# Attention outputs of units 4 to 23: their stores to HBM issued from ScalarE's queue in place of SyncE's

## The reference, cut to what matters

```python
def _attn_ref(q, k, v, alpha):               # batch 4, heads 8, seq 768, dim 48
    for t in range(S):
        state = alpha[:, :, t, :, None] * state + einsum('bhd,bhe->bhde', k[:, :, t], v[:, :, t])
        y[:, :, t] = einsum('bhd,bhde->bhe', q[:, :, t], state)

def _moe_ref(x, w_in, w_out):                # 3072 tokens, d_model 384, d_ff 2048
    h = x @ w_in
    return (h * (1.0 / (1.0 + np.exp(-1.702 * h)))) @ w_out

def _moe2_ref(x, w_in, w_out):               # the same sizes
    h = x @ w_in
    return (h - np.tanh(h)) @ w_out
```

## Time and profile before

| | |
|---|---|
| three runs | 967.51, 967.76, 970.03 us; median 967.76 |
| the profiled execution, its own time | 967.3 us |
| its span, first to last instruction | 965.5 us |
| granted TensorE clock, mean | 1.000 |
| busy: PE / DVE / ACT / POOL | 943.8 / 672.2 / 376.4 / 285.4 us |
| stores `attn_out<-y` from SPq | 92 of 48 KB, 1.8 us from issue to landing (median) |

### The profile page before, as it was taken

One profiled execution on the slowest core, in us unless ns is written; L12 is line 12 of the kernel. 1 busy time (PEld: TensorE's weight loads), 2 busy tenths in 40 slices (PEclk: granted clock), 3 DMA queues, 4 the chain that ended last, 5 costly groups with the idle time before them and its releaser, 6 DMA issues.

```text
span 965.5 us, 23370 instructions
## 1 busy us (share of the span) xinstructions
PE 943.8 (98%) x9705; PEld 830.0 (86%) x9705; DVE 672.2 (70%) x1615; ACT 376.4 (39%) x730; POOL 285.4 (30%) x314
## 2 busy tenths in 40 slices
PE   5899999999999999999999999999999999999998
PEld 4789999999999988888888888888888888888886
DVE  7879997878888877776322544357677677776765
ACT  1352333332332332333234664244444444444442
POOL 2666665646556554444001642000000000000000
PEclk9999999999999999999999999999999999999999
DMA  7943232423323332321113322010020020100101
GB/s 156 256 89 91 49 86 51 114 49 85 80 61 83 90 69 47 104 47 25 19 58 123 98 82 90 1 37 30 1 66 2 1 66 1 40 27 1 34 1 33
DMA packets 136234, 58.94 MB, mean 61 GB/s; under 512 B 114368, under 2 KB 131520, under 8 KB 136128
## 3 DMA queue, kind: packets, MB, share of 16 engines
q1 hardware_dynamic: 133488, 55.39, 22.8%
q10 hardware_dynamic: 2640, 2.05, 0.7%
HBM read 43.26 MB, written 13.96 MB: 59 GB/s over the span
## 4 chain that ended last, share of the span: by engine, by line
PE 92%; DVE 3%; DMA 2%; SPq 1%; POOL 1%; issue 1%; ACT 0%; DVEq 0%; POOLq 0%; ACTq 0%
PE pX L840 39%; PE pZ L864 16%; PE pX L864 9%; PE pZ L908 6%; PE pZ L914 6%; PE pX L908 4%; PE pX L704 3%; PE pZ L799 2%; PE pZ L732 2%; PE pZ L690 1%; PE pZ L742 1%; DMA k<-k_t 1%; PE pX L835 1%; PE pX L718 1%; PE pZ L790 1%; DVE scores L1212 1%
## 5 line engine op out<-in xcount | busy, mean ns | idle before, releaser
L840 PE MATMUL pX<-x_hi,w_hi 128*128 128x512 f32 (+2 forms) x624 | 227.7, 365 | 0.7 <-ACT g L1050 0.7
L840 PE MATMUL pX<-x_lo,w_hi 128*128 128x512 f32 (+2 forms) x624 | 227.3, 364 | 0.0
L840 PE MATMUL pX<-x_hi,w_lo 128*128 128x512 f32 (+2 forms) x624 | 227.3, 364 | 0.0
L1228 DVE TENSOR_TENSOR g_lo<-g,g_hi 128x512 fp32r<-128x512 f32 (+2 forms) x208 | 129.3, 637 | 87.5 <-ACT g_hi L1059 87.3
L1059 ACT ACTIVATE g_hi<-g 128x512 fp32r<-128x512 f32 (+2 forms) x208 | 121.3, 583 | 89.5 <-DVE g L1308 85.9
L1050 ACT ACTIVATE g<-pX 128x512 f32<-128x512 f32 (+3 forms) x144 | 65.7, 456 | 206.4 <-PE pX L840 173.2
L1308 DVE TENSOR_TENSOR g<-pX,sg 128x512 f32<-128x512 f32 x96 | 66.3, 690 | 106.2 <-ACT sg L1052 106.2
L840 PEld LDWEIGHTS pX<-x_hi,w_hi 128*128 128x128 f32 x624 | 117.5, 188 | 18.0 <-ACT g L1050 1.1
L840 PEld LDWEIGHTS pX<-x_lo,w_hi 128*128 128x128 f32 x624 | 117.5, 188 | 16.9
L840 PEld LDWEIGHTS pX<-x_hi,w_lo 128*128 128x128 f32 x624 | 117.5, 188 | 16.8
L596 POOL TENSOR_TENSOR r<-r,alpha 112x128 f32<-112x128 f32 (+2 forms) x115 | 109.5, 968 | 18.5 <-DMA r<-q_t 14.9
(11 more groups left out here) (166 smaller groups left out, 1899.4 us busy)
## 6 DMA issues: line engine op xcount, KB each, us to landing
v<-v_l SPq DMA_DIRECT2D x96, 48.0 KB, 2.6
x_raw<-hidden SPq DMA_DIRECT2D x6, 768.0 KB, 5.7
attn_out<-y SPq DMA_DIRECT2D x92, 48.0 KB, 1.8
out_t<-o SPq DMA_DIRECT2D x10, 384.0 KB, 3.5
alpha<-a_t SPq DMA_DIRECT2D x24, 128.0 KB, 2.9
r<-q_t SPq DMA_DIRECT2D x24, 128.0 KB, 3.0
k<-k_t SPq DMA_DIRECT2D x24, 128.0 KB, 3.0
w_raw<-w_in SPq DMA_DIRECT2D x16, 192.0 KB, 2.4
```

Of the source, the lines that this page charges most:

```text
L840: last = nc.tensor.matmul(pH(N)[:, 0:w], win(wp, f, m), XS[T % 2][xp][:, m, 0:w], start=(n == 0), stop=(n == len(terms) - 1))
L1228: nc.vector.tensor_tensor(at(GLs, N), g_raw(N), at(GHs, N).bitcast(F32), ALU.subtract).then_inc(gl_done, 1)
```

## The change

The SP loop keeps its wait and its stores only up to iteration 4 (units 1 to 3). From unit 4 on, ScalarE, having copied the second item of a unit, waits for that copy to have been written and issues the four stores itself. The waits of the other queues are unchanged. 80 of the 92 stores move, in 20 units. In the SP loop the values' load of unit U+1 now stands behind its own wait for `y_done` alone.

```diff
+        FROM_SP = 4
+
         def store_y(eng, U, batches=U2):
...
                 if U == 1:
                     sp.wait_ge(y_copied, 1)
                     first_inputs(sp, ((0, 0), (0, 1), (1, 0), (1, 1)))
-                sp.wait_ge(y_copied, 2 * U)
+                if U <= FROM_SP:
+                    sp.wait_ge(y_copied, 2 * U)
                 if U == 1:
                     first_inputs(sp, ((2, 0), (3, 0)))
-                else:
+                elif U <= FROM_SP:
                     store_y(sp, U - 1)
...
                 nc.scalar.activation(Y[U % 2][:, :, 2 * pp:2 * pp + 2, :], pY[buf(j)].rearrange("d (z q) t -> d z q t", z=2),
                                      ACT.Copy).then_inc(y_copied, 1)
+                if pp and U >= FROM_SP:
+                    act.wait_ge(y_copied, j + 1)
+                    store_y(act, U)
```

## The result

The changed kernel takes **980.25 us** (median; 978.87 to 981.96 over four runs) beside 968.89 us for the kernel before (967.51 to 970.03). The ratio is **1.0122, 95% interval 1.0108 to 1.0137**: 11.8 us slower by the ratio (the medians themselves lie 11.4 us apart). In a second comparison on another occasion it was 980.33 beside 968.47 us, 1.0123 (1.0098 to 1.0147). The forecast was 978 us, in a range of 969.5 to 986.

What follows compares the result with a forecast made beforehand. TensorE was taken to bound the kernel, its waits for the gelu adding 3.4 + 2.9 + 2.6 + 0.2 + 0.8 + 0.1 = 10.0 us to 967.8, so 978 us. The range was 969.5 to 986.

Steps and rivals of the forecast that it cites:

- What bounds the kernel: From unit 4 on TensorE always has work; faster loads or stores give back about 1 us at most, its waits add time.
- ScalarE is held by its issues: Ahead of the gelu, ScalarE stands idle for the whole length of its four issues, about 2.4 us in 20 units.
- D + 0.24 - room: TensorE's wait at odd items: D is the four issues' length, room the gelu-to-up(N+1) gap, 1.19 to 2.56 us; sum 10.0 us.
- D taken from SP's rows: ScalarE's four issues last as long as SP's did, unit by unit: 1.78 us at least, 2.65 to 3.02 in others.
- long ones: Sets of four store issues of 2.65 to 3.02 us instead of 1.78; twelve of the 20 units expected.
- q8 packet: A packet moved by the instruction queue within a unit's issues; long issues go with it, 1.78 us ones have none.
- Sharing with SP's queue: SP's values' loads run beside ScalarE's stores and lengthen issues by 0 to 7%, at most 1.5 us in all.
- The cover of VectorE and GpSimd: A later g_hi delays VectorE and GpSimd but is hidden, costed at nothing; without more cover 6 us, for the range.
- Rival 1: The prolonging sits in SP's sequencer; ScalarE issues in 1.78 us, leaving 2 us, 969.8 us in all; chance 0.15.
- Rival 2: SP's values' issues go between ScalarE's in 13 units: 23 us more, 33 in all, 1001 us; chance 0.08.
- Rival 3: With SP free, transfers come early and remove waits: at most 1.3 us gained, 967 us; chance 0.04.

Runs made afterwards that it cites:

- Experiments 1: The changed kernel, with ScalarE issuing the four stores behind g_hi of the same visit instead of ahead of the gelu: 970.63 us, 1.0017 of the kernel before.
- experiment 2: The kernel before, plus only ScalarE's wait for its own copy of y in the 20 units; SP still stores: 968.83 us, 0.9998 of the kernel before.
- experiment 6: The changed kernel measured once more, unchanged: 980.33 us, 1.0123 of the kernel before.
- experiment 5: The changed kernel, with each unit's output in eight stores of 24 KB instead of four of 48 KB: 1034.26 us, 1.0681 of the kernel before.
- experiment 4: The changed kernel, with ScalarE issuing two of a unit's four stores and SP the other two: 969.10 us, 0.9995 of the kernel before.
- experiment 7: The changed kernel, with ScalarE issuing two of each unit's four stores ahead of the gelu and two behind g_hi: 970.18 us, 1.0015 of the kernel before.

## Why the prediction was right, point by point

- **What bounds the kernel.** Right. SP now waits in other places (86.7 us for stores to land, where it waited 9.4), and nothing came of it, neither gain nor loss.
- **ScalarE is held by its issues.** Right: 44.9 us of idle put down to "issue" in 18 visits, 2.5 us each, against the 2.4 forecast. Experiments 1 and 2 separate it from ScalarE's queue as such and from the wait for the copy.
- **D + 0.24 - room.** Right in form, and its two hand-overs of 0.05 us are those of the chain above. Too small by 0.1 us at each of 14 visits: TensorE loses that beyond its wait. Of the 2.0 us between 10.0 forecast and 12.0 found, this is about 1.6, and other lengths D make the rest. The constant is the term of the sum that was mis-sized.
- **D taken from SP's rows.** Right on the whole: 20 units took 48.9 us on ScalarE, after 48.2 on SP. Each of the 11 long ones (2.48 us and more) again has a q8 packet that starts within it, and the eight in which none starts are at 1.79 to 2.25. Which units are hit is nearly the same as before: item 43 dropped out, item 9 came in (with a packet, but short). The place moves from run to run, the sum hardly. Item by item the agreement is in part luck: with the D of after, the 256 and 384 wide visits come out 1.1 us above the forecast and the 512 wide ones 0.9 us below. That no packet moved within a short one holds by the packets' starts alone: at items 17 and 23 one that had started earlier was still under way for 0.4 and 0.3 us of SP's issues.
- **Sharing with SP's queue.** Forecast as 0 to 7%, which was too little: it is 15% for most of the short ones, 0.27 us, and 26% at item 21. It matters only where the room is exceeded. There the issues under 0.7 us were longer than alone by 1.1 us in sum (1.4 in experiment 6), which is still under the 1.5 us that the range allowed; what sharing adds to a long issue can't be told apart.
- **The cover of VectorE and GpSimd.** Right. Over the same part of the program VectorE's waits for g_hi rose from 22.3 us (95 to 488 us before) to 45.4 (95 to 500 after), and TensorE's for scores fell. Even in experiment 5, with ScalarE late by 4 to 5 us, the profile has no wait of TensorE for scores, since TensorE was itself late.
- **Rival 1, the long issues are SP's own.** Fallen: ScalarE's are lengthened too.
- **Rival 2, one after another.** Fallen: 2.06 us beside SP's, not 3.7. With it falls, for this kernel, the reading that a whole issue locks the other queue out, which the Trainium skill ("Perfetto Trace Analysis", section "DMA Instruction — HWDGE (DVE, Sync)") suggests by its exclusive lock: the two queues' issues of 2.06 and 2.58 us ran over the same 2.7 us, where one after another they would take 4.4 (1.79 + 2.58). That a lock is held for a part of each issue is not excluded.
- **Rival 3, a gain.** Nothing of it in any run: the best of the variants, experiments 2 and 4, equal the kernel before. No version faster than the kernel before came out of this, and rows 1 and 2 say why: 1.3 us was all there was to gain.

What remains open is why an issue is longer when a q8 packet falls into it. In every trace each store issue over 0.8 us overlaps a packet of an instruction queue, on both queues, but for the first store of unit 1, which took 1.2 to 1.7 us without one. No run took the packet away, so that its part in this is not shown.

## What to carry to other kernels

Issuing a DMA occupies the queue that issues it, and the busy time doesn't show it: before moving DMAs to a compute engine, take the length of the issues from the DMA rows and compare it with the room between the end of the next instruction on that engine and its consumer. What fitted in the room was free here, what didn't was paid in full on every visit, with 0.1 us on top. Where the issues must be on that engine, put them behind the instruction that the bottleneck waits for; one place further down in ScalarE's program took the price from 11.8 to 1.6 us. Look also at what waits for the stores to land: in experiments 1 and 7 a load behind them came late, and TensorE waited 1.1 and 1.5 us for it at one visit. It was the number of issues that counted, not their bytes (453 ns at 24 KB, 466 at 48 KB).
